# Routing the tokens inside the FFN groups, with the fullest expert's weights and first tile prepared in the last group

## What is computed

```python
x = attention(q, k, v)                      # (2304, 512), all heads of a token side by side
gate = 1 / (1 + exp(-(x @ w_gate)))         # w_gate, w_val: 512 x 1536
y = (gate * (x @ w_val)) @ w_out            # w_out: 1536 x 512
logits = y @ moe2_w_gate                    # 512 x 8
expert_idx = argmax(logits, axis=1)
gate_w = softmax(logits)[arange(N), expert_idx]
for e in range(8):
    mask = expert_idx == e                  # skipped if empty
    h = maximum(y[mask] @ w1[e], 0)         # w1[e]: 512 x 1024
    out[mask] = gate_w[mask] * (h @ w2[e])  # w2[e]: 1024 x 512
```

## Time and profile before

| | |
|---|---|
| time before, median of 3 runs | 978.27 us (975.5 to 981.69) |
| the profiled execution | 973.81 us, its span 972.1 us |
| PE busy | 911.6 us (94%) |
| DVE, ACT, POOL busy | 334.3, 298.6, 259.1 us |
| granted PE clock, mean | 0.977 |
| tiles of the expert stage | 20 |

### The profile page before, as it was taken

How to read it: one execution, slowest core, us unless ns; L and a number is a source line. 1 busy time by engine, 2 the same in 40 slices (tenths; PEclk the granted TensorE clock), 3 DMA queues, 4 the chain that set the end, 5 groups by cost and what they waited for, 6 DMA issues and landing times.

```text
span 972.1 us, 15476 instructions
## 1 busy us (share of the span) xinstructions
PE 911.6 (94%) x5370; PEld 756.6 (78%) x5371; DVE 334.3 (34%) x634; ACT 298.6 (31%) x653; POOL 259.1 (27%) x251
## 2 busy tenths in 40 slices
PE   7999988999999999999999999998389999999995
PEld 3544444589999999999999999997368877888884
DVE  5767776731211201200210120112663454235421
ACT  5555554532321211212212122112253353134310
POOL 4133324411211111111111111110454364125421
PEclk9999999999999999999999999999599999999998
DMA  4544454422200100100000000000484466116310
GB/s 142 157 151 155 160 176 154 140 96 76 65 33 1 33 1 33 34 1 33 5 29 33 1 1 33 1 1 33 162 283 148 137 217 197 43 62 218 103 43 29
DMA packets 45541, 83.14 MB, mean 86 GB/s; under 512 B 6831, under 2 KB 19119, under 8 KB 45488
## 3 DMA queue, kind: packets, MB, share of 16 engines
q1 hardware_dynamic: 39728, 67.21, 21.2%
q0 software_dynamic: 3360, 10.49, 3.2%
q10 hardware_dynamic: 2400, 4.72, 1.3%
HBM read 68.17 MB, written 14.75 MB: 85 GB/s over the span
## 4 chain that ended last, share of the span: by engine, by line
PE 79%; DMA 7%; issue 5%; DVE 3%; POOL 2%; ACT 1%; SPq 1%; DVEq 0%; POOLq 0%; ACTq 0%
PE bank L1175 22%; PE bank L1177 22%; PE bank L1176 22%; DMA rinv_scratch<-rinv 3%; PE bank L1147 3%; PE bank L1108 3%; PE bank L1120 3%; DMA rwide<-rinv_scratch 2%; PE bank L1322 2%; PE bank L1234 2%; POOL ew1l L371 1%; DVE nmax L860 1%; DMA stage<-in_we 1%; PE bank L1225 1%; PE bank L1296 1%
## 5 line engine op out<-in xcount | busy, mean ns | idle before, releaser
L1175 PE MATMUL bank<-xh,w1h 128*128 128x384 f32 x576 | 196.2, 341 | 0.0
L1177 PE MATMUL bank<-xh,w1l 128*128 128x384 f32 x576 | 193.3, 336 | 0.0
L1176 PE MATMUL bank<-xl,w1h 128*128 128x384 f32 x576 | 193.1, 335 | 0.0
L589 POOL TENSOR_TENSOR hl<-hraw,hh 128x384 fp32r<-128x384 f32 x72 | 77.1, 1071 | 396.6 <-ACT hh L719 396.6
L905 DVE TENSOR_TENSOR hraw<-sig,bank 128x384 f32<-128x384 f32 x72 | 39.9, 554 | 347.1 <-ACT sig L748 347.1
L748 ACT ACTIVATE sig<-bank 128x384 f32<-128x384 f32 x72 | 35.4, 491 | 262.8 <-PE bank L1177 262.8
L1175 PEld LDWEIGHTS bank<-xh,w1h 128*128 128x128 f32 x576 | 108.3, 188 | 1.9
L1176 PEld LDWEIGHTS bank<-xl,w1h 128*128 128x128 f32 x576 | 108.3, 188 | 1.7
L1177 PEld LDWEIGHTS bank<-xh,w1l 128*128 128x128 f32 x576 | 108.1, 188 | 0.0
L690 ACT ACTIVATE prob<-bank,nmax 128x576 f32<-128x576 f32 (+2 forms) x144 | 75.9, 528 | 88.0 <-DVE nmax L860 85.6
L1177 PE MATMUL bank<-woh,hl 128*128 128x512 f32 x216 | 85.5, 396 | 0.0
(11 more groups left out here) (149 smaller groups left out, 1290.7 us busy)
## 6 DMA issues: line engine op xcount, KB each, us to landing
stage<-in_we SPq DMA_DIRECT2D x56, 512.0 KB, 4.4
w1raw<-in_w SPq DMA_DIRECT2D x8, 768.0 KB, 4.9
kt<-in_kT SPq DMA_DIRECT2D x16, 288.0 KB, 3.4
qt<-in_qT SPq DMA_DIRECT2D x16, 288.0 KB, 3.7
rwide<-rinv_scratch SPq DMA_DIRECT2D x32, 144.0 KB, 3.0
xt_scratch<-xo SPq DMA_DIRECT2D x16, 288.0 KB, 2.2
xraw<-xt_scratch SPq DMA_DIRECT2D x6, 768.0 KB, 5.3
y_scratch<-yrow ACTq DMA_DIRECT2D x6, 768.0 KB, 3.5
```

What stands on the lines that cost most here:

```text
L589: pool.tensor_tensor(hl[:, f % 2, :], hraw[:, f % 2, :], hh[:, f % 2, :].bitcast(F32), ALU.subtract).then_inc(h_low, 1)
L1175: pe.matmul(out_, wh, ah, start=first, stop=False, skip_group_check=True)
L1176: pe.matmul(out_, wh, al, start=False, stop=False, skip_group_check=True)
L1177: return pe.matmul(out_, wl, ah, start=False, stop=last, skip_group_check=True)
```

## The change

Three things are changed together.

1. The routing of a group is done inside the next group. `turn_y` moves to steps 3, 4, 5 and `router` to 4, 5, 6. In steps 4 and 5 the router product of one tile now stands directly ahead of the transposes of the next, and both use the same PSUM half. DVE then runs `routes`, `gates` and `slots` over 3 x 8 values per partition (22 small operations), PE the ranks (`ranks`, 6 matmuls of 8 to 24 columns, step 7), and in steps 9 to 11 one product of 432 columns per tile (`table`), whose sum DVE adds into a table in SBUF (`add_table`). A token's place is now a slot of its expert's own 18 columns, so it doesn't depend on the other experts' counts. The gates come from the sigmoid instead of Exp. The loops over groups are written out.

2. After group 3 is routed (in group 4), `first_expert` takes the expert with most tokens so far and `first_rows` the rows of its first tile. In the last group SP loads this expert's slices into three buffers, and ACT, DVE and POOL split them, from step 4 on. The w1 layout is changed so that the slices can lie in the parts of w1 that are no longer read. POOL gathers the first tile in step 1, PE transposes it in step 8. The expert stage then begins with this expert, the others follow in order.

3. After the last group PE runs the first tile (`expert_up`, `turn_hidden`, `expert_down`) while DVE routes the last group and then makes the tables of rows, of loads and of columns. The gather of tile 1 waits for the table of rows (`second_known`), the loads of the second expert for `loads_known`, the gather of tile 2 for `column_table` (`tables` at 2). From there `over_loads` begins with tile 1. Each gather and each `columns` on POOL first loads a register from `coltab`.

```diff
+    G_LAST, G_FIRST = NG - 1, NG - 3
...
-        YT_STEP, LG_STEP = [4, 6, 8], [5, 7, 9]
+        YT_STEP, LG_STEP = [3, 4, 5], [4, 5, 6]
+        HOT_STEP, RANK_STEP = 6, 7
+        TAB_STEP = [9, 10, 11]
+        ROWS0_STEP = 8
+        EW_STEP = 4
...
+            sp.wait_ge(first_known, 1)
+            sp.wait_ge(wo_low, FC)
+            sp.wait_ge(x_low, NG)
+            sp.wait_ge(gv_done, FC * G_LAST)
             load(0)
+            sp.wait_ge(loads_known, 1)
...
+                    col = pool.value_load(coltab[0:1, bass.ds(t, 1)], min_val=0, max_val=NCOL - 1)
+                    pool.tensor_copy(gcol[:], gidx[:, bass.ds(col, 1)]).then_inc(gcol_done, 1)
...
+            pool.wait_ge(second_known, 1)
+            pool.wait_ge(ygT_done, 1)
+            pool.wait_ge(y_stored, 16 * NG)
+            gather(1)
+            pool.wait_ge(tables, 1)
+            columns(0)
+            pool.wait_ge(tables, 2)
+            gather_ahead(0)
+
             def first_step(l, par, t):
                 if isinstance(l, int) and l == 0:
-                    columns(0)
                     gather_ahead(t)
+                    scatter(t)
+                    pool.wait_ge(out_stored, 16 * t)
+                    columns(t)
                     weights_low(pool, l + 1, 1 - par, LOW_POOL, ew_low_p)
                     return
...
+            hidden(0)
+            rows_high(1)
+            act.wait_ge(loads_known, 1)
             over_loads(act, first_step, lambda l, par, t: hidden(t))
...
+            def spread(G, m):
+
+                i = GM * G + m
+                if i:
+                    dve.wait_ge(table_done, i)
+                done(dve.tensor_tensor(a1h[:], iota_c[:], shl[:, 0, m:m + 1].to_broadcast([P, NCOL]), ALU.is_equal))
+                done(dve.tensor_tensor(b1h[:], iota_c[:, 0:P], shl[:, 1, m:m + 1].to_broadcast([P, P]), ALU.is_equal), 1)
+                for a, x in ((0, ids1[:, i:i + 1]), (1, gateh[:, m:m + 1].bitcast(F32)), (2, gatel[:, m:m + 1].bitcast(F32))):
+                    done(dve.tensor_tensor(ag[:, a * NCOL:(a + 1) * NCOL], a1h[:], x.to_broadcast([P, NCOL]), ALU.mult),
+                         0 if a == 2 else 1)
...
+            dve.sem_inc(orow_done, 1)
+            hidden(0)
+            row_table()
+            load_table()
+            slot_tables()
+            rows_low(1)
+            column_table()
+            dve.wait_ge(loads_known, 1)
             over_loads(dve, first_step, lambda l, par, t: hidden(t))
...
+            def ranks(G):
+
+                pe.wait_ge(rstep, ONEHOT[G])
+                hot = oneh[:].rearrange("p m e -> p (m e)")
+                pe.matmul(rank_psum, ltri_r[:], hot, start=True, stop=False, skip_group_check=True)
+                pe.matmul(rank_psum[:, E:], ones_r[:], hot[:, 0:(GM - 1) * E], start=False, stop=False,
+                          skip_group_check=True)
+                pe.matmul(rank_psum[:, 2 * E:], ones_r[:], hot[:, 0:E], start=False, stop=True, skip_group_check=True)
+                for m in range(GM):
+                    last = pe.matmul(cnt_psum, ones_r[:], hot[:, m * E:(m + 1) * E], start=(m == 0), stop=(m == GM - 1),
+                                     skip_group_check=True)
+                last.then_inc(ranks_done, 1)
...
-            pe.wait_ge(rpool, 2)
-            for t in range(TT):
-                if t % (TT // HOT_PARTS) == 0:
-                    pe.wait_ge(rstep, R_HOT + t // (TT // HOT_PARTS))
-                last = pe.matmul(bank[1][:, 0, 0:3 * NTAB], b1h[:, t, :], ag[:, t, :], start=(t == 0),
-                                 stop=(t == TT - 1))
-            last.then_inc(rmm, 1)
...
-            turn_rows(0)
+            expert_up(0, 0, 0)
+            turn_hidden(0)
+            table_last()
+            expert_down(0, 0, 1)
+            turn_rows(1)
+            pe.wait_ge(loads_known, 1)
             over_loads(pe, first_step, step)
```

798 lines of the change are left out of this document (487 added, 311 removed).

## The result

| | before | after |
|---|---|---|
| time, median of 20 runs each, side by side | 978.8 us (973.9 to 982.28) | 973.29 us (968.28 to 977.54) |
| ratio | | 0.9948, 95% interval 0.9931 to 0.9966 |
| span of the profiled execution | 972.1 us | 969.7 us |
| PE busy | 911.6 us | 914.7 us |
| DVE busy | 334.3 us | 391.9 us |

The changed kernel is 5.5 us faster, 0.5%, with an interval of 3.3 to 6.8 us. The forecast was 976.3 us in a range of 971 to 982, 1.9 us less than before. So the time lies in the range and the direction is right, but the saving is nearly three times the one forecast, and the forecast's 1.9 lies outside the interval.

What follows compares the result with a forecast made beforehand. PE was taken as the bound, busy 94% of the span, with savings only in one thin stretch after the FFN. Profiled 973.81 + 10.9 - 12.8 = 971.9, on the median's scale 976.3 us, range 971 to 982.

Steps and rivals of the forecast that it cites:

- Inside the groups, +10.9: Five FFN groups: ranks, table products and two handoffs add 2.1 us each; with first tile's transposes +10.9, between 9.5 and 12.
- The rival of hidden or doubled handoffs: PE's waits on DVE's logits copy in the groups vanish or double: -4 or +4 us, inside the forecast's range.
- DVE's chains in the groups cost nothing: Routing on DVE inside the FFN groups priced at nothing, since DVE is busy for 1.97 us of 13.87.
- not ready in time: First tile's slices or rows are late, it starts at 10 rather than 4: +6, 982 us; chance 0.10.
- PE's own work in the tail runs at full clock until the first long wait: After the last group, first tile's up priced at 5.5 us plus 0.7 for ranks, down from 14.8 to 20.3.
- the slower rival: PE's clock stays at 1.2 GHz from the tail's first wait to its last: +13, 989 us; chance 0.13.
- The register load on POOL, 0.8: Ahead of each gather in the tail, POOL's register load costs 0.8 us, bounds 0 and 1.0.
- Gather 2 lands 4.6 us after its issue: Tile 2's rows, gathered amid weight slices, land at 32.5 us after the last group; PE idles over 3, dip costs 1.2.
- The second expert's slices hold ACT's ReLU until 51.8: Tile 2's hidden transposes wait from 47.4 to 51.8 us after the last group: 4.4 us and a second clock dip.
- The faster rival: Tile 2's ReLU wait vanishes, tile 4's row transposes come 51 to 52 us after the last group: 967 us; chance 0.22.
- The tail, -12.8: From the last group's end (zero) to tile 4's row transposes (the mark): 60.2 us instead of 73.0.
- Everything behind runs alike: After the transposes of tile 4's rows, before and after take the same time: difference 0.

Runs made afterwards that it cites:

- the last kernel: Changed kernel with router products between up and down and the second expert's slices split earlier on ACT, DVE and POOL: 964.28 us, 0.9872 of the kernel before.

## Why the prediction held, and where its steps did not

The number held with some luck. The range was 11 us wide and holds a change of nothing as well, and the forecast saving of 1.9 us was measured as 5.5.

- **The bound.** Right. PE has no idle time inside the groups but the handoffs, so each added us was paid in full, and the saving came out of the one thin stretch.
- **Inside the groups, +10.9.** Measured +10.4. The handoffs, 0.8 per group, are 0.85 by experiment; the table's 0.6 is 0.59; the ranks' 0.7 were mis-sized and are about 0.55, as the remainder says. The rival of hidden or doubled handoffs is out.
- **DVE's chains in the groups cost nothing.** Right: 3.3 us more busy time per two steps and no idle PE.
- **The first tile ready in time.** Right: up starts at 4.06. The rival "not ready in time" (mark later by 6) was right in its mechanism and too cheap, since late weights cost 12.1, of which 8.4 are waits and 3.7 the clock.
- **PE's own work in the tail runs at full clock until the first long wait.** This step failed. The clock fell in the first up, with PE busy since zero, and again in the first down. Up took about 8 us for 6.2, down 7.4 for 5.5, and the end of down came 4.1 us late, of which the two dips are about 3.2 (1.6 each, against the same passes at full clock). The trace of before had the sign: its clock was at 0.50 one us behind the router. The forecast put its 0.78 down to waits of 9 us. It is not the slower rival, which had the clock low from the first wait to the last; the mean of the tail is 0.92.
- **The register load on POOL, 0.8.** 1.05 us from `gidx` to the copy that follows, against 0.15 before, so 0.9; near the upper bound. It cost little, since gather 1 landed before PE was free.
- **Gather 2 lands 4.6 us after its issue and leaves over 3 us of wait and a dip.** Too high: 3.56, 1.82 us of wait, no dip. Together with PE's delay ahead of it this took back 2.8 of the 4.1 us. The Trainium skill, "DMA: Bandwidth & Descriptors", section "Anatomy of one DMA — SWDGE (gpsimd) path", gives an estimate of 2.6 us for such a gather; no awaited gather here is as low: they took 3.2 to 3.7 us with few slices in flight and 5.2 to 5.8 among them. That the prediction's estimate of about 973 us by this figure comes so near to the measured 973.29 is therefore chance.
- **The second expert's slices hold ACT's ReLU until 51.8.** Right, at 52.6, and it is the step on which the sum rests. Of the early lag only what comes through DVE and gather 3 reaches this chain of slice 1, slice 3, slice 7 and ReLU: where the first dip was missing, the transposes began at 50.9. So two errors nearly cancel, the dip that the forecast didn't have and the wait for gather 2 that it had too long. From the scatter's issue to the end of the columns the forecast had 4.4 us, and it is 4.0.
- **The faster rival** (without that wait the mark stands at 51 to 52) was a rival to keep, and the price was wrong: with the wait gone, the gathers are late and the mark is at 57.56, and at 56.32 in the last kernel.
- **The tail, -12.8.** -12.3 against the profile used, about -13.5 against three profiles of the kernel before. That its tail varies by 2.3 us with the clock the forecast didn't say; its range was wide enough for it.
- **Everything behind runs alike.** In work yes, in time no: one dip of the clock at expert 4 is missing, 1.1 us.

The sum: +10.4 - 13.5 - 1.3 = -4.4 us with three profiles before (226.83, 226.99, 227.25 behind the mark), inside the measured 3.3 to 6.8. The forecast's -1.9 is off by 0.7 in what the tail saves, 0.5 inside the groups, and 1.3 for that dip.

## What to carry to other kernels

Before moving work off a thin stretch onto a full engine, look for what ends the stretch's waits: here the routing moved into the groups was only worth its 10 us because the weights were made ready too, and what ended the new tail was the order in which POOL works off slices, a scatter's landing and gathers. Where two products share a PSUM half through another engine's copy, put any other work of PE between them; here that was 4 us for three moved lines. Compare stages rather than whole times when a stage is steadier than the whole (here the FFN, within 0.15 us), and profile the kernel before more than once. Split a stage into PE's busy and idle time before calling an edit without effect: a lower clock in one profile can hide what an edit took off the waits, and a higher one can pass for it.

## What the runs showed of the hardware

- The clock fell to 0.57 to 0.63 in the first up with PE busy for the 4.06 us ahead of it, all of them on narrow products, in six profiles of eight with that order and no products added behind the router. In the kernel before it was at 0.50 one us behind the same work. The Trainium skill, "TensorE: Matmul & The Clock Gate", section "What's actually happening", tells of a halved clock after PE was idle; these rows show it where it was busy. That the narrow products bring it is argued, not shown.
- Behind a wait of about 3.2 us at the same place of the program the clock fell in seven profiles and stayed in six. It also fell behind a wait of 2.06 us, in one profile.
- A gather of 256 KB landed after 3.56 us when issued 4.5 us behind the last of four slice loads, and after 5.2 us when issued 1.7 us behind it. Issuing it 2.7 us sooner brought its rows 1.1 us sooner.
- A register load from SBUF on POOL costs about 0.9 us ahead of the instruction that needs it.
- A handoff from PE to DVE and back through one PSUM half cost 0.42 us, of which the copy is 0.17.
